# Attention and expert layer on one core: the first two head pairs' loads on GpSimd's queue, the first pair's split behind the last relu, identity products on TensorE

## The reference, cut to what matters

```
scores = q @ k.T / sqrt(64)                       # 4 batches, 8 heads, 576 tokens, head size 64
x      = log1p(|i - j|) / log1p(max(i, 1))
bias   = relu(x * w1 + b1) @ w2                   # 32 hidden units, one value per head, all i and j
attn   = softmax(scores + bias)
y      = attn @ v                                 # 2304 tokens of 512
e[s]   = argmax(y @ w_gate) if s == 0 or sigmoid(y @ w_local) < 0.5 else e[s - 1]
out    = softmax(y @ w_gate)[e] * relu(y @ W1[e]) @ W2[e]        # 8 experts, 512 -> 1024 -> 512
```

## Time and profile before

| | |
|---|---|
| Median of 3 runs | 767.16 us (765.99 to 768.0) |
| Profiled execution, own time | 767.78 us, of which the profile's span is 766.0 |
| TensorE busy in the span | 659.5 us (86%) |
| VectorE, ACT, GpSimd busy | 389.0, 345.8, 197.8 us |
| Constants land | about 7.6 us |
| Bias stage | 8.5 to 74 us |
| First scores of pair 0 and of pair 1 | 74.2 and 91.0 us |
| Attention ends, experts begin | about 370 and 425 us |
| Busy share of the DMA engines, 0 to 20 us | 0.33, 88 GB/s |

### The profile page before, as it was taken

The page is one execution under the profiler, slowest core; times in us unless marked ns, Lnnn a source line. Parts: engine busy times, 40 slices in busy tenths (PEclk is TensorE's granted clock), DMA queues, the critical chain, the costliest instruction groups (busy, mean ns, idle before and its releaser), DMA issues.

```text
span 766.0 us, 13200 instructions
## 1 busy us (share of the span) xinstructions
PE 659.5 (86%) x4323; PEld 525.8 (69%) x4323; DVE 389.0 (51%) x785; ACT 345.8 (45%) x707; POOL 197.8 (26%) x171
## 2 busy tenths in 40 slices
PE   4776899999999999999404599998899999999994
PEld 1222788788888888887204477886778878888883
DVE  5997575556566555555596134248442442222220
ACT  4895666565666665565210233255522341222211
POOL 2000614444444544440171011111211111112101
PEclk9999999999999999999755689999999999999999
DMA  3996644444444444440560734143611111111100
GB/s 85 211 227 160 136 92 95 95 93 102 101 94 95 94 97 100 98 94 17 191 263 7 268 124 151 41 151 127 237 41 41 41 34 41 41 41 41 41 14 0
DMA packets 68184, 77.05 MB, mean 101 GB/s; under 512 B 46767, under 2 KB 47279, under 8 KB 68144
## 3 DMA queue, kind: packets, MB, share of 16 engines
q1 hardware_dynamic: 63392, 64.58, 32.4%
q0 software_dynamic: 4080, 11.54, 4.7%
q10 hardware_dynamic: 672, 0.44, 0.2%
HBM read 69.06 MB, written 11.27 MB: 105 GB/s over the span
## 4 chain that ended last, share of the span: by engine, by line
PE 68%; DVE 12%; ACT 8%; issue 5%; DMA 3%; ACTq 2%; SPq 1%; DVEq 0%; POOL 0%; POOLq 0%
PE ps_pv L1210 15%; PE ps_s L1188 15%; PE ps_pv L1111 11%; PE ps_s L1040 7%; DVE hid L751 4%; PE ps_t L1064 4%; PE ps_t L1086 3%; ACT sm L590 3%; PE ps_s L1052 3%; PE ps_x L1125 3%; PE ps_s L1199 2%; DMA bias<-stage 2%; PE ps_s L1020 1%; DVE w1lo L950 1%; DVE w2lo L950 1%
## 5 line engine op out<-in xcount | busy, mean ns | idle before, releaser
L765 DVE CUSTOM_DVE_ANT_0 sm<-ps_s,bias 128x576 f32<-128x576 f32 x128 | 91.7, 754 | 70.7 <-PE ps_s L1040 70.7
L590 ACT ACTIVATE sm<-sm,negmax 128x576 f32<-128x576 f32 x144 | 111.9, 778 | 3.7 <-DVE negmax L765 3.7
L1210 PE MATMUL ps_pv<-w2hi,hThi 128*128 128x512 f32 x200 | 81.1, 405 | 9.0 <-DVE w2lo L950 7.7
L977 DVE TENSOR_TENSOR hTlo<-ps_s,hThi 128x512 fp32r<-128x512 f32 x50 | 32.2, 686 | 105.6 <-ACT hThi L699 105.6
L1210 PE MATMUL ps_pv<-w2hi,hTlo 128*128 128x512 f32 x200 | 78.8, 394 | 0.0
L1210 PE MATMUL ps_pv<-w2lo,hThi 128*128 128x512 f32 x200 | 78.7, 393 | 0.0
L1111 PE MATMUL ps_pv<-pT,vt 128*64 128x320 f32 (+1 forms) x512 | 69.1, 410 | 4.7 <-issue 1.0
L1188 PE MATMUL ps_s<-w1hi,xThi 128*128 128x512 f32 x200 | 66.1, 412 | 8.1 <-DVE w1lo L950 6.7
L706 ACT ACTIVATE ysb<-ps_pv,pcur 128x512 f32<-128x512 f32 x25 | 17.2, 688 | 122.7 <-PE ps_pv L1210 109.4
L538 POOL DMA_INDIRECT out_dram<-ysb,sidx x25 | 25.3, 1011 | 179.3 <-ACT ysb L706 167.8
L487 POOL CAST ksplit<-raw 128x1152 fp32r<-128x1152 f32 x15 | 17.2, 1147 | 204.7 <-DMA raw<-in_kq_dram 204.6
(11 more groups left out here) (187 smaller groups left out, 1337.7 us busy)
## 6 DMA issues: line engine op xcount, KB each, us to landing
w1raw<-in_moe_w_dram SPq DMA_DIRECT2D x18, 1024.0 KB
w2raw<-in_moe_w_dram SPq DMA_DIRECT2D x18, 1024.0 KB
raw<-in_kq_dram SPq DMA_DIRECT2D x32, 432.0 KB, 5.3
bias<-stage SPq DMA_DIRECT2D x32, 288.0 KB, 4.7
raw<-in_kq_dram SPq DMA_DIRECT2D x32, 128.0 KB, 5.0
vt<-in_v_dram SPq DMA_DIRECT2D x32, 128.0 KB, 2.5
tokens_dram<-xl SPq DMA_DIRECT2D x64, 64.0 KB, 1.8
bias_tail<-stage SPq DMA_DIRECT2D x4, 144.0 KB, 2.5
```

The costliest lines, as they stand in the source:

```text
L590: nc.scalar.activation(probs, probs, ACT.Exp, scale=-1.0, bias=negmax[:, u % 2, hd:hd + 1], accum_out=sums[:, pr % 2, 2 * t + hd:2 * t + h ...
L765: nc.vector.tensor_tensor_reduce(sm[:, u % 2, S * hd:S * (hd + 1)].rearrange("p (a c) -> p a c", a=2), ps_s[:, hd, :, 0:HALF], bias.rearra ...
L977: V.tensor_tensor(hTlo[:, 4 * i:4 * i + 4, :].rearrange("p k t -> p (k t)"), ps_s[:, 1, i, :], hThi[:, 4 * i:4 * i + 4, :].bitcast(F32).re ...
L1210: last = nc.tensor.matmul(ps_pv[:], h[:, f, :], w[:, f, :], start=f == 0 and h is hThi and w is w2hi, stop=f == KF - 1 and h is hTlo)
```

## The change

w1s and b1s are loaded by GpSimd instead of ACT, with a semaphore of their own. The loads of pairs 0 and 1 and of the gates leave SP's queue: GpSimd issues pair 0's and the gates' 12 DMAs when its tables are filled, and pair 1's 10 DMAs when VectorE has done 24 of the 36 steps, and it starts the split of pair 1 behind that of pair 0. VectorE splits pair 0 behind the last step instead of two steps ahead of it, with the low part of k ahead of that of q, and clears two corners of ps_pv at the start. TensorE runs eight products of the identity with itself when ident is made and eight more behind the shift, and the first scores wait for the high parts and the low part of k first and for the low part of q later.

```diff
-        CONSTS = 16 * (G + G + 2)
+        CONSTS = 16 * (G + G)
...
+        def load_qk_part(queue, pr, half, part):
+            s, kqb = pr % 2, kq[pr // PAIRS, pr % PAIRS]
+            landed = raw_first[s] if pr < 2 else raw_in[s]
...
+        def load_v_half(queue, pr, half):
+            s = pr % 2
+            landed = v_first[s] if pr < 2 else v_in[s]
...
@@ sync: the loop of the steps
-                if m == 5:
-                    sp.wait_ge(zeroed, 10)
-                if 6 <= m < 6 + 3 * 2 * PARTS and m % 3 == 0:
-                    load_qk_part(0, (m - 6) // 3 // PARTS, (m - 6) // 3 % PARTS)
-                if m in (28, 29):
-                    load_v_half(0, m - 28)
-                if m in (31, 32):
-                    load_gates(m - 31)
-            load_qk(1)
-            load_v(1)
@@ gpsimd
             pool.sem_inc(y_left, LEAD)
+            nc.gpsimd.dma_start(w1s[:], w1c).then_inc(w1_small, 16)
+            nc.gpsimd.dma_start(b1s[:], b1c).then_inc(w1_small, 16)
             nc.gpsimd.memset(w2bd[:], 0.0).then_inc(zeroed, 1)
...
-            pool.wait_ge(hid_ready, LEAD + STEPS)
+            pool.wait_ge(zeroed, 10)
+            for half in range(2):
+                for part in range(PARTS):
+                    load_qk_part(nc.gpsimd, 0, half, part)
+            for half in range(2):
+                load_v_half(nc.gpsimd, 0, half)
+                load_gates(nc.gpsimd, half)
+            pool.wait_ge(hid_ready, LEAD + STEPS - 12)
+            for half in range(2):
+                for part in range(PARTS):
+                    load_qk_part(nc.gpsimd, 1, half, part)
+            for half in range(2):
+                load_v_half(nc.gpsimd, 1, half)
+            pool.wait_ge(qk_ready, 2)
             split_pair(1)
@@ scalar
-            nc.scalar.dma_start(w1s[:], w1c).then_inc(consts_in, 16)
-            nc.scalar.dma_start(b1s[:], b1c).then_inc(consts_in, 16)
@@ vector
+            nc.vector.memset(ps_pv[D:P, 0:TAIL], 0.0).then_inc(corners, 1)
+            nc.vector.memset(ps_pv[0:D, 2 * P + TAIL:2 * P + 2 * TAIL], 0.0).then_inc(corners, 1)
             dve.wait_ge(consts_in, CONSTS)
+            dve.wait_ge(w1_small, 32)
...
-                dve.wait_ge(raw_in[0], 96)
+                dve.wait_ge(raw_first[0], 96)
                 nc.vector.tensor_copy(ksplit[:, 0], raw[:, 0, 0:2, :]).then_inc(hi_split, 1)
                 nc.vector.tensor_copy(qh, raw[:, 0, 2:4, :]).then_inc(hi_split, 1)
                 dve.wait_ge(hi_split, 2)
-                nc.vector.tensor_tensor(ql, raw[:, 0, 2:4, :], qh.bitcast(F32), ALU.subtract).then_inc(qk_ready, 1)
                 nc.vector.tensor_tensor(ksplit[D:P, 0], raw[D:P, 0, 0:2, :], ksplit[D:P, 0].bitcast(F32),
                                         ALU.subtract).then_inc(qk_ready, 1)
+                nc.vector.tensor_tensor(ql, raw[:, 0, 2:4, :], qh.bitcast(F32), ALU.subtract).then_inc(qk_ready, 1)
             for m in range(STEPS):
...
-                if m == STEPS - 3:
-                    split_first_pair()
-            nc.vector.memset(ps_pv[D:P, 0:TAIL], 0.0).then_inc(corners, 1)
-            nc.vector.memset(ps_pv[0:D, 2 * P + TAIL:2 * P + 2 * TAIL], 0.0).then_inc(corners, 1)
+            split_first_pair()
@@ tensor
+            def ident_products(n):
+                for _ in range(n):
+                    nc.tensor.matmul(ps_t[:, 0, 0:P], ident[:], ident[:], start=True, stop=True)
+            pe.wait_ge(zeroed, 6)
+            ident_products(8)
             pe.wait_ge(w2_in, 16 * G)
-            pe.wait_ge(consts_in, CONSTS)
+            pe.wait_ge(w1_small, 32)
...
             last.then_inc(shift_made, 1)
+            ident_products(8)
...
-                if t == 0:
+                if u == 0:
+                    pe.wait_ge(hi_split, 2)
+                    pe.wait_ge(qk_ready, 1)
+                elif t == 0:
                     pe.wait_ge(qk_ready, 2 * pr + 2)
...
                         for part in (qhi, qlo):
+                            if u == 0 and part is qlo:
+                                pe.wait_ge(qk_ready, 2)
```

More of the change, by code:

```diff
@@ L204, in build @@
         v_in = [sem(f"v_in{i}") for i in range(2)]
+        raw_first = [sem(f"raw_first{i}") for i in range(2)]
+        v_first = [sem(f"v_first{i}") for i in range(2)]
+        w1_small = sem("w1_small")
         hi_split = sem("hi_split")
@@ L304, in load_window, with load_gates @@
                                     ap=[[NCOL, C], [C * NCOL, G], [1, NCOL - G + 1]])).then_inc(consts_in, 16)
+        def load_gates(queue, half):
+            rows = slice(D * half, D * (half + 1))
+            c0 = HW * half + D
+            queue.dma_start(turn[rows, :, c0:c0 + NL],
+                              wg.rearrange("(r two d) e -> two d r e", two=2, d=D)[half]).then_inc(turn_in, 16)
+        def load_qk_part(queue, pr, half, part):
+            s, kqb = pr % 2, kq[pr // PAIRS, pr % PAIRS]
+            landed = raw_first[s] if pr < 2 else raw_in[s]
+            rows = slice(D * half, D * (half + 1))
+            if part == 0:
+                queue.dma_start(raw[rows, s, 0:3, :], kqb[:, 0:3, :]).then_inc(landed, 16)
+            elif part == 1:
+                queue.dma_start(raw[rows, s, 3, TAIL:S], kqb[:, 3, 0:P * FULL]).then_inc(landed, 16)
+            else:
+                queue.dma_start(raw[rows, s, 3, 0:TAIL], kqb[:, 3, P * FULL:S]).then_inc(landed, 16)
+        def load_v_half(queue, pr, half):
+            s = pr % 2
+            landed = v_first[s] if pr < 2 else v_in[s]
+            vb = v[pr // PAIRS, :, P * (pr % PAIRS):P * (pr % PAIRS + 1)]
+            cols, k0, k1 = slice(D * half, D * (half + 1)), TAIL * half, P * FULL * (1 - half)
+            queue.dma_start(vt[:, s, 0:FULL, cols],
+                              vb[k0:k0 + P * FULL, cols].rearrange("(k p) c -> p k c", p=P)).then_inc(landed, 16)
+            queue.dma_start(vt[cols, s, FULL, cols], vb[k1:k1 + TAIL, cols]).then_inc(landed, 16)
         def bias_rows_in(t):
@@ L317, in _ @@
                 nc.sync.dma_start(w2bd[C * g:C * (g + 1), H * g:H * (g + 1)], w2).then_inc(w2_in, 16)
-            def load_gates(half):
-                rows = slice(D * half, D * (half + 1))
-                c0 = HW * half + D
-                nc.sync.dma_start(turn[rows, :, c0:c0 + NL],
-                                  wg.rearrange("(r two d) e -> two d r e", two=2, d=D)[half]).then_inc(turn_in, 16)
-            def load_qk_part(pr, half, part):
-                s, kqb = pr % 2, kq[pr // PAIRS, pr % PAIRS]
-                rows = slice(D * half, D * (half + 1))
-                if part == 0:
-                    nc.sync.dma_start(raw[rows, s, 0:3, :], kqb[:, 0:3, :]).then_inc(raw_in[s], 16)
-                elif part == 1:
-                    nc.sync.dma_start(raw[rows, s, 3, TAIL:S], kqb[:, 3, 0:P * FULL]).then_inc(raw_in[s], 16)
-                else:
-                    nc.sync.dma_start(raw[rows, s, 3, 0:TAIL], kqb[:, 3, P * FULL:S]).then_inc(raw_in[s], 16)
             def load_qk(pr):
@@ L338, in load_qk @@
                     for part in range(PARTS):
-                        load_qk_part(pr, half, part)
-            def load_v_half(pr, half):
-                s = pr % 2
-                vb = v[pr // PAIRS, :, P * (pr % PAIRS):P * (pr % PAIRS + 1)]
-                cols, k0, k1 = slice(D * half, D * (half + 1)), TAIL * half, P * FULL * (1 - half)
-                nc.sync.dma_start(vt[:, s, 0:FULL, cols],
-                                  vb[k0:k0 + P * FULL, cols].rearrange("(k p) c -> p k c", p=P)).then_inc(v_in[s], 16)
-                nc.sync.dma_start(vt[cols, s, FULL, cols], vb[k1:k1 + TAIL, cols]).then_inc(v_in[s], 16)
+                        load_qk_part(nc.sync, pr, half, part)
             def load_v(pr):
@@ L352, in load_v @@
                 for half in range(2):
-                    load_v_half(pr, half)
+                    load_v_half(nc.sync, pr, half)
             def save_pair(pr):
@@ L480, in split_pair @@
                 s = pr % 2
-                pool.wait_ge(raw_in[s], 96 * (pr // 2 + 1))
+                if pr == 1:
+                    pool.wait_ge(raw_first[1], 96)
+                else:
+                    pool.wait_ge(raw_in[s], 96 * (pr // 2))
                 if pr >= 2:
@@ L1095, in values @@
                 if g == 0:
-                    pe.wait_ge(v_in[s], 64 * (pr // 2 + 1))
+                    pe.wait_ge(v_first[s] if pr < 2 else v_in[s], 64 * max(1, pr // 2))
                 pe.wait_ge(copied_a, u + 1)
```

## The result

The changed kernel took 772.54 us (median of 4 runs, 771.06 to 772.95) against 767.12 us for the kernel before on the same chip: ratio 1.0068, 95% interval 1.0049 to 1.0087. It is slower by 5.2 us, where 4.8 us of gain was forecast. The profiled execution after took 771.06 us (span 769.3), the fastest of its four, and the one before was 0.6 us above its median. So the two traces show only 3.3 us of the difference (769.3 less 766.0), and the ratio carries the verdict.

The account below looks back on a forecast made before the run. TensorE's products bound the kernel from 95 us on; ahead of them VectorE's relus, with the DMA engines a near second. Terms 1.0 + 1.9 - 2.4 - 1.3 + 3.8 + 1.8 = 4.8 us gain: 762.4 us, range 758.0 to 769.0.

Parts of the forecast that it names:

- e: End of the relus: last relu to first add_bias shrinks from 8.64 to 4.85 us, a gain of 3.8 us.
- f: Pair 1: its load and split come earlier, so TensorE's wait ahead of pair 1 goes, a gain of 1.8 us.
- Term c: Second pair's loads issued behind step 24, where DMA is 0.99 busy: a stall costing 2.4 us, bounds 0 and 6.6.
- the loads starve the stores: Rival: the second pair's loads cost the whole 6.6 us instead of 2.4; gain 0.6, 766.6 us; chance 0.15.
- Term b: First pair's loads leave SP's queue, so VectorE's waits for late bias stores in the relus go: a gain of 1.9 us.
- Term a: Start: earlier constants and identity products raising TensorE's clock, less 0.8 us for tail stores: a gain of 1.0 us.
- Term d: VectorE beside GpSimd: twelve DMA issues take 0.11 us each from the relus, a cost of 1.3 us.
- rival two: GpSimd's 22 issues hold VectorE's relus: slower, 780.2 us at the full 0.977 us each; chance 0.11.
- h: Price of each GpSimd issue beside relus: gain is 8.5 - 22h, zero at 0.39 us.
- Rival three: VectorE's back-to-back relus shut GpSimd out, so pair 0's loads wait for the last relu: 770.4 us; chance 0.04.

Follow-up runs that it names:

- split_moved: The kernel before with only the split of the first pair moved behind the last relu, no load or queue changed: 762.75 us, ratio 0.9930.
- best_w1_pool: Changed kernel without the sixteen identity products, pair 0's loads on SP behind w2bd's, pair 1's behind the last store, w1s and b1s on GpSimd: 760.07 us.
- p1_paced: Changed kernel with pair 1's ten loads still on GpSimd, but one behind each third step's relus from 9 to 30: 766.64 us, 0.9987 of the kernel before.
- best_final: Changed kernel; w1s, b1s on ACT; pair 0's loads on SP behind w2bd's, pair 1's among stores; nine late identity products replace the sixteen: 762.57 us.

## Why the prediction was wrong

**The two terms behind the relus were right.** e and f were forecast at 3.8 and 1.8, 5.6 together; split_moved gained 5.4. In the trace e is 3.4 and f 2.1, less 1.3 for the clock, so that 5.4 meets 5.6 so closely is partly luck. (The addends of e sum to 4.76, not 4.85; 5.20 was measured.) Two steps of it were wrong all the same. I put f down to the loads' new queue, but it follows from the split's place. And I let "products with qhi already run while qlo is made" stand without a look at the clock that TensorE's 1.47 and 0.79 us pauses would bring: 1.3 us longer behind it. The 0.61 of the earlier trace rows behind the old split was the warning.

**Term c was mis-sized.** The rest of the change was forecast at -0.8 us and measured at -10.6 (+5.2 less -5.4). The largest part is the burst: 2.4 forecast, 5.6 us of waits measured, and 8.1 us by the run without it, drain and slower relus included. The step that failed is the subtraction of 1.5 us of spare bandwidth and 2.1 us of slack. The slack was computed from the shortest landing, 3.2 us, for stores that now took up to 11.0. And what counts is one store that lands 7.7 us late amid the burst (52.71 to 63.64 us), with TensorE and VectorE idle for most of it, not the bytes that would fit beside all stores. The bound that I had from the bytes, 6.6 us, was nearly the value. This was my rival "the loads starve the stores", at 0.15; its time of 766.6 was too low, as it left the other terms as they were.

**Term b gave nothing.** The waits between 27 and 48 us did vanish, as forecast. But pair 0's loads now met the tail stores, whose landing went from a median of 2.5 to 5.3 us (the 144 KB ones), and 2.5 us of waits came back at 24 us. I had the collision in view ("the pair's loads now run beside them") and priced it at part of 0.8 us.

**Term a was nearly nothing.** The first relu came 0.6 us sooner, and w1s and b1s on GpSimd are worth about 1.0 us by best_w1_pool. The identity products started at 5.09 us, where I had them (5.15), but at "at most 0.22 us each" they took 0.47. The price came from a row of transposes, which show as one record each, and a product with ident shows as two: per record it took 0.24 us. So the first eight lasted to 8.87 us, past the landing of w2bd, the second eight to 10.95 instead of 9.8, and they pushed step 0's products back, which start at 9.96 without them. (The profile's clock row reads 1.00 from 5 to 9 us, although eight more took only 2.05 us just behind them.) Step 2's relus still waited 0.92 us, against 0.98, and step 3's began at 14.06 us, where I had 12.6 and the kernel before 14.41.

**Term d was about right in size, by luck.** Forecast 1.3, measured 1.6 us from the mean of 592 against 577 ns. I had the same small price for each of twelve issues and nothing for the other ten. The trace has relus beside the twelve longer by 1.0 us in all and beside the ten by 0.6, and 1.1 of this lies beside the four large issues of v (L331), which held a relu for 0.23 to 0.28 us each. So rival two was right in kind and wrong in size: h is 0.07 us on average, and 0.39 would have eaten the gain. Rival three fell: the issues took 0.53 to 0.83 us beside relus that ran back to back. The Trainium skill (SBUF — State Buffer, "SBUF: two separate sides") says that a DMA from GpSimd can't write its descriptors while VectorE runs a two-port operation, and that the one of the two that starts first blocks the other. The trace agrees that they hold each other up (a relu of 0.86 us beside an issue of v), but GpSimd was never kept out for longer than a relu: an issue of raw took 0.53 to 0.59 us beside relus (once 0.81) and 0.56 us in VectorE's pause before 12.20. Whether the relu is such an operation no view tells.

**A term was missing.** GpSimd's closing drain, 2.0 us for 24 more DMAs. Nothing at the end of the kernel was part of my sum, as I read the views only where the diff touches.

The account by the traces: waits 5.9, relus 1.6, first relu -0.6, behind the last relu -3.4, low clock 1.3, pair 1 -2.1, drain 2.0, together 4.7 us slower, near the 5.2 measured. The profiled pair itself differs by 3.3, since a stage that the change doesn't touch ran 1.4 us faster in the one execution profiled.

## What to carry to other kernels

Where the DMA engines are near full beside a paced loop, look for the place at which they idle and load there: 20 us at 0.33 busy took all of pair 0's loads at no cost. Among the stores the same bytes cost about their own transfer time in waits if they come in a burst (5.6 us from GpSimd's queue, 6.5 from SP's), and about a third of it if spread (1.9 us by the time of p1_paced, some 2 us of waits in best_final). Before a wait is credited to a transfer's place, ask what its queue was waiting for: moving one 4.2 us job behind a loop moved the next loads too and gained 5.4 us, where all the rest of the change lost 10.6.

## What the runs showed of the hardware

GpSimd's drain at the program's end grows with the number of DMAs that it issued, whatever their size and however long before: 4.230 us in the kernel before, 4.397 with 2 more, 5.213 with 12, 5.377 with 14 and 6.193 with 24, which is 0.082 us for each, on the path of every run. GpSimd's large issues of v (0.79 to 0.83 us) made the relu beside them take 0.81 to 0.86 us instead of 0.58, and an issue of raw added at most 0.06. Twenty-four transfers of half a kilobyte beside the relus came with 2.3 us more of VectorE's waits, far beyond their bytes. And an f32 product of 128x128 by 128x128 with ident took 0.47 us at the start and, a few microseconds later, 0.26 to 0.39 us from one execution to the next (2.05 to 3.10 us for eight).
